# Routing between an attention and its experts: first row fetch moved into the attention's program, a weight split moved ahead, extra identity transposes on TensorE

## Chip, core and metric

The kernel runs on one core of one Trainium2 chip. The metric is device time in microseconds (us), the median of several executions. Engines: TensorE (PE in the profile; PEld is its weight load), VectorE (DVE), ScalarE (ACT), GpSimd (POOL) and SyncE (SP).

## What is computed

An attention over 4 x 12 heads of 448 tokens feeds a layer of 8 experts in which every token goes to one expert only, and that feeds a dense gated layer:

```python
x = attention(q, k, v, g_q, g_k)                  # 1792 tokens x 768
logits = (x / (|x| + 1e-6)) @ en.T / tau          # en: normed embeddings of 8 experts
expert_idx = np.argmax(logits, axis=1)
gate_w = softmax(logits)[arange, expert_idx]
for e in range(8):
    mask = expert_idx == e
    out[mask] = gate_w[mask, None] * (relu(x[mask] @ w1[e]) @ w2[e])
return (sigmoid(out @ w_gate) * (out @ w_val)) @ w_out
```

## The kernel before

The kernel is three programs in a row: `attention`, `experts` and `layer2`. Each is a block in which every engine has a list of instructions of its own in the order written, with semaphores between engines. [...]

**Routing, the end of the attention.** Tokens lie in 16 tiles of 112 rows (`TILES`); 12 are "early" (the first three batches), 4 are "late". For the late tiles VectorE picks the best expert (`best`), TensorE counts with two small products (`count`), and VectorE's `ranks` turns the counts into a slot for each token: prefix sum, subtract, add, mask, reduce, and four small steps that give the slot's chunk `r.a` and its line `r.b`. `chunk_of(i)` and `line_of(i)` write one-hot matrices HI and LO for tile i, and `index_map` multiplies LO by HI on TensorE, in all 16 products that add up in one bank: the token number of every slot. VectorE then copies that bank to `c.index` (the rows of the first job), `c.indices` (all rows, as integers) and `c.tokens` (the same as floats). In between it finishes the gates: GpSimd raises the squared norms to the power 0.5 (L520), VectorE adds 1e-6, inverts, scales the logits, ScalarE takes the exponential, and SyncE writes the gates to DRAM beside x (`write_gate`, L314).

**Experts.** Work is cut into jobs of up to 294 tokens of one expert. A job fetches its rows by three indirect DMAs of 98 rows from GpSimd (`fetch_rows`, parts a = 0, 1, 2), multiplies them by their gates (`scale_rows` on VectorE for a = 0 and 2, `scale` on ScalarE for a = 1), turns them on TensorE into six banks, and splits them into a high and a low part, XH by ScalarE and XL by VectorE (`x_out`). Each layer product is then three products (high x high, low x high, high x low). `h(j, f)` is block f of the hidden layer, 18 products; its weight block needs its low part W1L from VectorE (`w1_split`), whose high part W1H comes from ScalarE. There are two buffers, so W1H of block f can only be written when h of block f - 2 is done. W1H of blocks 0 and 1 is made already in the attention's program. Before its first job, VectorE also computes the table of jobs (`job_table`, L1444 to L1470), clears the ends of six banks, copies the turned slot table for SyncE (`tokens_T`, L1476), and, after the six `x_out`, makes the low parts of seven weight slots of layer 2 (L1512).

Of the kernel before, what the change touches and what calls it, by code (L numbers as in the profile page):

```python
# [22 lines left out]
F32 = mybir.dt.float32  # L23
# [8 lines left out]
NT = 4  # L32
# [6 lines left out]
E = 8  # L39
# [144 lines left out]
def attention(nc, c, q, k, v, g_q, g_k, emb, tau, w1, w2, w_l2, w_sums, x_rows):  # L184
# [5 lines left out]
    with ExitStack() as ctx:  # L190
# [208 lines left out]
        def _(pool):  # L399
# [120 lines left out]
            nc.gpsimd.tensor_tensor(r.norm[:, EARLY:], r.ssq[:, EARLY:], r.half[:, EARLY:], ALU.pow).then_inc(r.norm_pow, 1)  # L520
        @block.vector
        def _(dve):
# [129 lines left out]
            def ranks(tiles, OH, mask, incl, place, before, rest, tot):  # L652
# [12 lines left out]
                chain(nc.vector.tensor_scalar(r.y[:, tiles], r.r[:, tiles], 1.0 / LINES, 0.5 / LINES - 0.5,  # L665
                                              ALU.mult, ALU.add))
                chain(nc.vector.tensor_scalar(r.y[:, tiles], r.y[:, tiles], ROUND, None, ALU.add))
                chain(nc.vector.tensor_scalar(r.a[:, tiles], r.y[:, tiles], ROUND, None, ALU.subtract))
# [22 lines left out]
            def early_ranks():  # L691

                dve.wait_ge(r.counted_e, 1)
                ranks(early, r.OHE, r.mask_e, r.incl_e, r.place_e, r.cap, tqk[:, 0:E * EARLY],
                      tqk[:, E * EARLY:2 * E * EARLY]).then_inc(r.ranked_e, 1)
                only(nc.vector.tensor_tensor(r.carry[:, :], r.cap[:, :], r.incl_e[:, :, EARLY - 1], ALU.add))
# [24 lines left out]
            def finish():  # L721
# [20 lines left out]
                ranks(late, r.OHL, r.mask_l, r.incl_l, r.place_l, r.carry, sc[1][:, 0, 0:E * NT],  # L742
                      sc[1][:, 0, E * NT:2 * E * NT]).then_inc(r.ranked_l, 1)
                dve.wait_ge(r.norm_pow, 1)
                chain(nc.vector.tensor_scalar(r.norm[:, late], r.norm[:, late], 1e-6, None, ALU.add))
                chain(nc.vector.reciprocal(r.norm[:, late], r.norm[:, late]))
                nc.vector.tensor_tensor(r.L[:, late, :], r.L[:, late, :],
                                        r.norm[:, late].unsqueeze(2).to_broadcast(over_e), ALU.mult).then_inc(r.exp_in, 1)
                dve.wait_ge(r.ranked_l, 1)
# [13 lines left out]
                nc.vector.tensor_copy(c.tokens[:, :], sc[0][0:ROWS, 1, 0:SLOTS]).then_inc(c.all_indices, 1)  # L763
# [104 lines left out]
        def _(pe):  # L868
# [190 lines left out]
            count(r.OHL, sc[1][:, 0, 0:E * NT], sc[1][:, 0, E * NT:2 * E * NT], E * NT, r.counted_l)  # L1059
            index_map(range(EARLY, TILES)).then_inc(r.mapped, 1)  # L1060
# [18 lines left out]
def fetch_rows(nc, c, x_rows):  # L1079

    for a in range(GATHERS):
        nc.gpsimd.indirect_dma_start(out=c.xr[:, a, :], out_offset=None, in_=x_rows[:, :],
                                     in_offset=bass.IndirectOffsetOnAxis(ap=c.index[:, a:a + 1], axis=0))\
            .then_inc(c.x_got[a], 16)
# [108 lines left out]
def experts(nc, c, w1, w2, w_l2, w_sums, x_rows, table_of_slots, ids):  # L1193
# [4 lines left out]
    with ExitStack() as ctx:  # L1198
# [22 lines left out]
        slots_written = sem("slots_written")  # L1221
        tokens_T = sb("tokens_T", [HALF, 2, LINES], U32)
# [115 lines left out]
        def _(pool):  # L1338
# [8 lines left out]
            for ring in range(2):  # L1347
                pool.wait_ge(c.x_written[ring], 16 * PAIRS // 2)
            pool.wait_ge(c.gate_written, 16 * B)
            pool.wait_ge(c.first_index, 1)  # L1350
            fetch_rows(nc, c, x_rows)
# [3 lines left out]
            pool.wait_ge(c.all_indices, 2)  # L1355
# [18 lines left out]
        def _(act):  # L1374
# [21 lines left out]

            for k in range(7):
                nc.scalar.activation(c.WH[:, k, :], first_slot(k), ACT.Copy).then_inc(c.w_hi, 1)
# [18 lines left out]
        def _(dve):  # L1417
# [55 lines left out]
            for bank in hb + yb:  # L1473
                nc.vector.memset(bank[:, TS:T], 0.0).then_inc(banks_set, 1)
            dve.wait_ge(tokens_turned, 2)
# [29 lines left out]
            for f in range(2):  # L1505
                w1_split(0, f)
            scale_rows(0, 2)
            for kd in range(KD):
                x_out(0, kd, first_banks[kd])
            for k in range(7):  # L1510
                dve.wait_ge(c.w_hi, k + 1)
                nc.vector.tensor_tensor(c.WL[:, k, :], first_slot(k), c.WH[:, k, :].bitcast(F32),  # L1512
                                        ALU.subtract).then_inc(c.w_lo, 1)
# [4 lines left out]
        def _(pe):  # L1518
# [48 lines left out]

            n_jobs = jobs(pe, pe.wait_ge)
            pe.wait_ge(banks_set, HB + YB)
            for part in range(2):  # L1570
                nc.tensor.transpose(hb[2][0:HALF, part * 128:part * 128 + LINES],
                                    c.tokens[0:LINES, part * HALF:(part + 1) * HALF],
                                    c.ident[0:LINES, 0:LINES]).then_inc(tokens_turned, 1)
            pe.wait_ge(tokens_out, 1)
            for a in range(GATHERS):
                pe.wait_ge((gated_dve, gated_act)[a % 2], a // 2 + 1)
                for kd in range(KD):
                    last = nc.tensor.transpose(first_banks[kd][:, a * R:(a + 1) * R], xr[0:R, a, kd * 128:(kd + 1) * 128],
                                               c.ident[0:R, 0:R])
                    if a == GATHERS - 1:  # L1580
                        last.then_inc(x_turned, 1)
# [539 lines left out]
```

## Time and profile before

| | us |
|---|---|
| median of 3 runs | 1154.52 (1153.01 to 1155.78) |
| the profiled execution's own time | 1155.25 |
| span of its trace | 1153.8 |

The trace is one execution. Its span starts with the first instruction; 1.45 us of the device time lie outside it. Times in the rows below are us from the span's start. [...] Busy time of TensorE says little about its speed, since a product at the low clock is busy for twice as long.

### The profile page before, as it was taken

To read this page: it belongs to the slowest core of one execution; us is meant where nothing else is said; L and a number is where in the kernel's file an instruction comes from. 1 tells how busy PE (TensorE), PEld (TensorE's weight loads), DVE (VectorE), ACT (ScalarE), POOL (GpSimd) and SP (SyncE) were. 2 spreads that over 40 slices of the span, in tenths; PEclk is the share of its full clock that TensorE was granted. 3 is DMA by queue.
4 is the path that set the end of the run, shared out by engine and by line. 5 is a ranking of instruction groups with operands and counts; after the bars stand their busy time and mean duration, and the time that the engine had idled before them with its cause. 6 is when DMAs were issued, how large, how long until landed. Compare 5 with 4: busy or idle time off the path is not lost. (4 is left out here: it accounts for less than half of the span.)

```text
span 1153.8 us, 21938 instructions
## 1 busy us (share of the span) xinstructions
PE 1104.7 (96%) x7312; PEld 978.3 (85%) x7313; DVE 779.7 (68%) x1416; ACT 597.4 (52%) x1414; POOL 365.0 (32%) x363
## 2 busy tenths in 40 slices
PE   7999999999959899999999899999999999999997
PEld 6566666666649899999999899999999999999997
DVE  5789988788677545565556796475568675574672
ACT  4777777777625555565555663242245343341441
POOL 7798887888421110111011501100003012000002
PEclk9999999999959999999999999999999999999999
DMA  4355565543427667786778433142231334331312
GB/s 124 90 154 146 171 197 142 150 118 104 130 66 200 162 188 180 189 220 170 183 196 218 120 104 102 50 123 76 82 111 56 110 99 150 108 104 48 111 42 96
DMA packets 207779, 149.64 MB, mean 130 GB/s; under 512 B 12446, under 2 KB 203550, under 8 KB 207718
## 3 DMA queue, kind: packets, MB, share of 16 engines
q1 hardware_dynamic: 203910, 133.80, 42.1%
q0 software_dynamic: 3568, 14.82, 4.2%
q8 instruction: 36, 0.59, 0.2%
q10 hardware_dynamic: 240, 0.23, 0.1%
q14 instruction: 25, 0.20, 0.1%
HBM read 128.29 MB, written 20.53 MB: 129 GB/s over the span
## 5 line engine op out<-in xcount | busy, mean ns | idle before, releaser
L1984 PE MATMUL qb<-BH,l_WH 128*128 128x448 f32 x504 | 185.9, 369 | 3.0 <-DVE BL L1854 3.0
L1986 PE MATMUL qb<-BH,l_WL 128*128 128x448 f32 x504 | 185.9, 369 | 0.0
L1985 PE MATMUL qb<-BL,l_WH 128*128 128x448 f32 x504 | 185.9, 369 | 0.0
L1689 ACT ACTIVATE l_WH<-stream 128x384 fp32r<-128x384 f32 x209 | 100.8, 515 | 127.4 <-PE ob L2007 102.4
L1925 POOL TENSOR_TENSOR quads<-quads 128x448 f32<-128x448 f32 x24 | 30.6, 1276 | 381.7 <-DVE quads L1793 381.7
L1793 DVE TENSOR_TENSOR quads<-qb,quads 128x448 f32<-128x448 f32 x168 | 100.1, 619 | 67.6 <-PE qb L1986 67.4
L1789 DVE TENSOR_TENSOR l_WL<-stream,l_WH 128x384 fp32r<-128x384 f32 x209 | 121.3, 599 | 20.4 <-ACT l_WH L1689 20.4
L791 ACT ACTIVATE PR<-sc,negmax 112x448 f32<-112x448 f32 x192 | 121.9, 658 | 0.7 <-DVE negmax L533 0.5
L1539 PE MATMUL hb<-XH,W1H 128*128 128x256 f32 (+1 forms) x384 | 112.7, 294 | 7.4 <-issue 4.0
L1539 PE MATMUL yb<-HH,W2H 128*128 128x256 f32 (+1 forms) x384 | 112.8, 294 | 0.4 <-DVE W2L L1480 0.4
L2005 PE MATMUL ob<-l_WH,GH 128*128 128x384 f32 x336 | 112.5, 335 | 0.4 <-DVE Y L1873 0.4
L533 DVE TENSOR_REDUCE negmax<-sc 112x2 f32<-112x896 f32 x96 | 100.6, 1085 | 17.6 <-PE sc L914 17.0
L2007 PE MATMUL ob<-l_WH,GL 128*128 128x384 f32 x336 | 112.3, 334 | 0.0
L2006 PE MATMUL ob<-l_WL,GH 128*128 128x384 f32 x336 | 112.2, 334 | 0.0
L1541 PE MATMUL hb<-XH,W1L 128*128 128x256 f32 (+1 forms) x384 | 111.7, 291 | 0.0
L1540 PE MATMUL hb<-XL,W1H 128*128 128x256 f32 (+1 forms) x384 | 111.5, 290 | 0.0
L1540 PE MATMUL yb<-HL,W2H 128*128 128x256 f32 (+1 forms) x384 | 109.8, 286 | 0.0
L1541 PE MATMUL yb<-HH,W2L 128*128 128x256 f32 (+1 forms) x384 | 109.7, 286 | 0.0
L1984 PEld LDWEIGHTS qb<-BH,l_WH 128*128 128x128 f32 x504 | 95.1, 189 | 12.3 <-issue 3.2
L1423 DVE TENSOR_TENSOR W1L<-raw,W1H 128x384 fp32r<-128x384 f32 x132 | 67.9, 556 | 51.9 <-ACT W1H L1379 43.7
L1986 PEld LDWEIGHTS qb<-BH,l_WL 128*128 128x128 f32 x504 | 95.0, 189 | 9.4
L1985 PEld LDWEIGHTS qb<-BL,l_WH 128*128 128x128 f32 x504 | 95.0, 189 | 9.1
(251 smaller groups left out, 2536.1 us busy)
## 6 DMA issues: line engine op xcount, KB each, us to landing
raw<-in_moe_w_dram SPq DMA_DIRECT2D x68, 384.0 KB, 5.1
stream<-in_moe_w_dram SPq DMA_DIRECT2D x48, 512.0 KB, 5.1
stream<-w_sums SPq DMA_DIRECT2D x92, 192.0 KB, 2.4
w_sums<-Sb SPq DMA_DIRECT2D x12, 768.0 KB, 6.3
stream<-in_moe_w_out_dram SPq DMA_DIRECT2D x48, 192.0 KB, 2.4
stream<-in_moe_w_val_dram SPq DMA_DIRECT2D x36, 192.0 KB, 3.0
stream<-in_moe_w_gate_dram SPq DMA_DIRECT2D x33, 192.0 KB, 2.6
raw<-in_q_dram SPq DMA_DIRECT2D x24, 224.0 KB, 3.3
```

Of the source, the lines that this page charges most:

```text
L791: nc.scalar.activation(PR[:, h, j, :], sc[j % 2][0:P, h, 0:S], ACT.Exp, bias=negmax[:, s, j, h:h + 1], accum_out=den[:, s, h, j:j + 1]).th ...
L1539: nc.tensor.matmul(out[:, 0:n], WH[:, slot, k, :], mh, start=(k == 0), stop=False)
L1540: nc.tensor.matmul(out[:, 0:n], WH[:, slot, k, :], ml, start=False, stop=False)
L1541: last = nc.tensor.matmul(out[:, 0:n], WL[:, slot, k, :], mh, start=False, stop=(k == blocks - 1))
L1689: nc.scalar.activation(W(c.WH, n), c.stream[:, n % RING, :], ACT.Copy).then_inc(c.w_hi, 1)
L1789: nc.vector.tensor_tensor(W(c.WL, n), c.stream[:, n % RING, :], W(c.WH, n).bitcast(F32), ALU.subtract).then_inc(c.w_lo, 1)
L1984: nc.tensor.matmul(bank, wh, bh, start=(k == 0), stop=False)
L1985: nc.tensor.matmul(bank, wh, bl, start=False, stop=False)
L1986: mm = nc.tensor.matmul(bank, wl, bh, start=False, stop=(k == 2))
L2005: nc.tensor.matmul(bank, GH[:, f, at], W(c.WH, slot), start=(f == 0), stop=False)
L2006: nc.tensor.matmul(bank, GH[:, f, at], W(c.WL, slot), start=False, stop=False)
L2007: mm = nc.tensor.matmul(bank, GL[:, f, at], W(c.WH, slot), start=False, stop=(f == 3))
```

## The change

- GpSimd's fetch of part 0 for job 0 moves from the start of the experts' program to the end of the attention's (`fetch_rows(..., range(1))`), with its waits for the written rows, gates and index. Parts 1 and 2 stay in the experts' program.
- In the late tiles' ranks, the three steps on the norms (add, reciprocal, multiply) stand between the rank steps instead of behind them.
- `c.tokens` is copied by ScalarE at the start of the experts' program, no longer by VectorE at the end of the attention's.
- On VectorE, W1L of block 0 and the low part of weight slot 0 stand ahead of the `tokens_T` copy, and slots 1 and 2 stand ahead of the six `x_out`.
- TensorE gets identity transposes that nobody reads (`keep_busy`): 24 ahead of the last four index products, 40 at the start of the experts' program, 6 behind the token transposes and 4 ahead of each part's row transposes.

```diff
@@ -518,6 +518,12 @@
             nc.gpsimd.tensor_scalar(gsum, gsum, 1e-9, None, ALU.add).then_inc(r.gsum_e, 1)
             pool.wait_ge(r.ssq_l, 1)
             nc.gpsimd.tensor_tensor(r.norm[:, EARLY:], r.ssq[:, EARLY:], r.half[:, EARLY:], ALU.pow).then_inc(r.norm_pow, 1)
+            for ring in range(2):
+                pool.wait_ge(c.x_written[ring], 16 * PAIRS // 2)
+            pool.wait_ge(c.gate_written, 16 * B)
+            pool.wait_ge(c.first_index, 1)
+            fetch_rows(nc, c, x_rows, range(1))
+
         @block.vector
         def _(dve):
             nc.vector.memset(power[:, :], -0.5).then_inc(fixed, 1)
...
@@ -662,10 +668,13 @@
                                               before[:, :].unsqueeze(2).to_broadcast(wide), ALU.add))
                 chain(nc.vector.tensor_tensor(place[:, :, :], place[:, :, :], OH[:, :, :], ALU.mult))
                 chain(nc.vector.tensor_reduce(r.r[:, tiles], place[:, :, :].rearrange("p e i -> p i e"), AX.X, ALU.add))
-                chain(nc.vector.tensor_scalar(r.y[:, tiles], r.r[:, tiles], 1.0 / LINES, 0.5 / LINES - 0.5,
-                                              ALU.mult, ALU.add))
-                chain(nc.vector.tensor_scalar(r.y[:, tiles], r.y[:, tiles], ROUND, None, ALU.add))
-                chain(nc.vector.tensor_scalar(r.a[:, tiles], r.y[:, tiles], ROUND, None, ALU.subtract))
+            def over_lines(tiles):
+
+                return nc.vector.tensor_scalar(r.y[:, tiles], r.r[:, tiles], 1.0 / LINES, 0.5 / LINES - 0.5,
+                                               ALU.mult, ALU.add)
+
+            def line_in_chunk(tiles):
+
                 return nc.vector.scalar_tensor_tensor(out=r.b[:, tiles], in0=r.a[:, tiles], scalar=-float(LINES),
                                                       in1=r.r[:, tiles], op0=ALU.mult, op1=ALU.add)
 
...
@@ -739,13 +752,17 @@
                 chain(nc.vector.tensor_tensor(r.L[:, late, :], r.LG[:, late, :],
                                               r.mx[:, late].unsqueeze(2).to_broadcast(over_e), ALU.subtract))
                 dve.wait_ge(r.counted_l, 1)
-                ranks(late, r.OHL, r.mask_l, r.incl_l, r.place_l, r.carry, sc[1][:, 0, 0:E * NT],
-                      sc[1][:, 0, E * NT:2 * E * NT]).then_inc(r.ranked_l, 1)
+                numbers(late, r.OHL, r.mask_l, r.incl_l, r.place_l, r.carry, sc[1][:, 0, 0:E * NT],
+                        sc[1][:, 0, E * NT:2 * E * NT])
                 dve.wait_ge(r.norm_pow, 1)
-                chain(nc.vector.tensor_scalar(r.norm[:, late], r.norm[:, late], 1e-6, None, ALU.add))
-                chain(nc.vector.reciprocal(r.norm[:, late], r.norm[:, late]))
+                only(nc.vector.tensor_scalar(r.norm[:, late], r.norm[:, late], 1e-6, None, ALU.add))
+                chain(over_lines(late))
+                only(nc.vector.reciprocal(r.norm[:, late], r.norm[:, late]))
+                chain(nc.vector.tensor_scalar(r.y[:, late], r.y[:, late], ROUND, None, ALU.add))
                 nc.vector.tensor_tensor(r.L[:, late, :], r.L[:, late, :],
                                         r.norm[:, late].unsqueeze(2).to_broadcast(over_e), ALU.mult).then_inc(r.exp_in, 1)
+                chain(nc.vector.tensor_scalar(r.a[:, late], r.y[:, late], ROUND, None, ALU.subtract))
+                line_in_chunk(late).then_inc(r.ranked_l, 1)
                 dve.wait_ge(r.ranked_l, 1)
                 chunk_of(EARLY).then_inc(r.hi_l, 1)
                 line_of(EARLY).then_inc(r.lo_l, 1)
@@ -760,7 +777,6 @@
                 dve.wait_ge(r.mapped, 1)
                 nc.vector.tensor_copy(c.index[:, :], sc[0][0:ROWS, 1, 0:GATHERS]).then_inc(c.first_index, 1)
                 nc.vector.tensor_copy(c.indices[:, :], sc[0][0:ROWS, 1, 0:SLOTS]).then_inc(c.all_indices, 1)
-                nc.vector.tensor_copy(c.tokens[:, :], sc[0][0:ROWS, 1, 0:SLOTS]).then_inc(c.all_indices, 1)
 
             sums(0, 0, 0)
             sums(0, 0, 1)
@@ -1057,6 +1073,7 @@
             index_map(range(EARLY // 2, EARLY))
             pe.wait_ge(r.picked_l, 1)
             count(r.OHL, sc[1][:, 0, 0:E * NT], sc[1][:, 0, E * NT:2 * E * NT], E * NT, r.counted_l)
+            keep_busy(sc[1][:, 1, :], 24)
             index_map(range(EARLY, TILES)).then_inc(r.mapped, 1)
 
 
...
@@ -1344,15 +1362,11 @@
                 nc.gpsimd.dma_start(ids[bass.ds(s, T), :].rearrange("(a l) o -> a (l o)", l=LINES),
                                     table_of_slots[bass.ds(slot, GATHERS), :]).then_inc(ids_out, 16)
 
-            for ring in range(2):
-                pool.wait_ge(c.x_written[ring], 16 * PAIRS // 2)
-            pool.wait_ge(c.gate_written, 16 * B)
-            pool.wait_ge(c.first_index, 1)
-            fetch_rows(nc, c, x_rows)
+            fetch_rows(nc, c, x_rows, range(1, GATHERS))
             n_jobs = jobs(pool, pool.wait_ge)
             pool.wait_ge(slots_written, 16)
             store_ids(0)
-            pool.wait_ge(c.all_indices, 2)
+            pool.wait_ge(c.all_indices, 1)
             with pool.Fori(0, n_jobs) as j:
                 pool.wait_ge(x_turned, KD * (j + 1))
                 pool.wait_ge(ids_out, 16 * (j + 1))
@@ -1394,6 +1408,8 @@
 
                 nc.scalar.activation(HH[:, f, :], hb[f % HB][:, 0:T], ACT.Relu).then_inc(h_hi, 1)
 
+            act.wait_ge(c.all_indices, 1)
+            nc.scalar.activation(c.tokens[:, :], c.indices[:, :], ACT.Copy).then_inc(tokens_copied, 1)
             for k in range(7):
                 nc.scalar.activation(c.WH[:, k, :], first_slot(k), ACT.Copy).then_inc(c.w_hi, 1)
             n_jobs = jobs(act, act.wait_ge)
@@ -1472,6 +1488,14 @@
             job_table()
             for bank in hb + yb:
                 nc.vector.memset(bank[:, TS:T], 0.0).then_inc(banks_set, 1)
+            w1_split(0, 0)
+
+            def slot_low(k):
+                dve.wait_ge(c.w_hi, k + 1)
+                nc.vector.tensor_tensor(c.WL[:, k, :], first_slot(k), c.WH[:, k, :].bitcast(F32),
+                                        ALU.subtract).then_inc(c.w_lo, 1)
+
+            slot_low(0)
             dve.wait_ge(tokens_turned, 2)
             nc.vector.tensor_copy(tokens_T[:, :, :], hb[2][0:HALF, 0:256].rearrange("p (h l) -> p h l", h=2)[:, :, 0:LINES])                .then_inc(tokens_out, 1)
             def w2_split(j, d, part):
@@ -1502,15 +1526,14 @@
                     scale_rows(j, a)
 
             scale_rows(0, 0)
-            for f in range(2):
-                w1_split(0, f)
+            w1_split(0, 1)
             scale_rows(0, 2)
+            slot_low(1)
+            slot_low(2)
             for kd in range(KD):
                 x_out(0, kd, first_banks[kd])
-            for k in range(7):
-                dve.wait_ge(c.w_hi, k + 1)
-                nc.vector.tensor_tensor(c.WL[:, k, :], first_slot(k), c.WH[:, k, :].bitcast(F32),
-                                        ALU.subtract).then_inc(c.w_lo, 1)
+            for k in range(3, 7):
+                slot_low(k)
             with dve.Fori(0, n_jobs) as j:
                 job_order(w1_split, w2_split, h_out, scale, x_out, lambda j, d: None, j)
 
@@ -1565,14 +1588,23 @@
                     if d + 1 < KD:
                         turn(j + 1, d + 1)
 
+            def keep_busy(bank, turns):
+
+                for _ in range(turns):
+                    nc.tensor.transpose(bank[:, 0:128], c.ident[:, :], c.ident[:, :])
+
+            keep_busy(tx[0], 40)
             n_jobs = jobs(pe, pe.wait_ge)
             pe.wait_ge(banks_set, HB + YB)
+            pe.wait_ge(tokens_copied, 1)
             for part in range(2):
                 nc.tensor.transpose(hb[2][0:HALF, part * 128:part * 128 + LINES],
                                     c.tokens[0:LINES, part * HALF:(part + 1) * HALF],
                                     c.ident[0:LINES, 0:LINES]).then_inc(tokens_turned, 1)
+            keep_busy(hb[0], 6)
             pe.wait_ge(tokens_out, 1)
             for a in range(GATHERS):
+                keep_busy(hb[0], 4)
                 pe.wait_ge((gated_dve, gated_act)[a % 2], a // 2 + 1)
                 for kd in range(KD):
                     last = nc.tensor.transpose(first_banks[kd][:, a * R:(a + 1) * R], xr[0:R, a, kd * 128:(kd + 1) * 128],
```

Where the instructions stand now, at three places.

TensorE at the end of the attention, from the fourth index product group to the barrier, before (sc0 holds the index bank, sc1 the counts):

```order
L1038 MATMUL sc0<-HI,LO 112x168 [waits hi_e1,lo_e] x6
L1023 MATMUL sc1<-OHL,tri 112x32 [waits picked_l]
L1024 MATMUL sc1<-OHL,ones 112x32
L1038 MATMUL sc0<-HI,LO 112x168 [waits hi_l,lo_l] x4
L190 UNCONDITIONAL_BRANCH
L1517 UNCONDITIONAL_BRANCH [waits barrier_Pool_Activation_PE_DVE_SP_release]
```

and of the change:

```order
L1054 MATMUL sc0<-HI,LO 112x168 [waits hi_e1,lo_e] x6
L1039 MATMUL sc1<-OHL,tri 112x32 [waits picked_l]
L1040 MATMUL sc1<-OHL,ones 112x32
L890 MATMUL sc1<-ident 128x128 x24
L1054 MATMUL sc0<-HI,LO 112x168 [waits hi_l,lo_l] x4
L190 UNCONDITIONAL_BRANCH
L1540 UNCONDITIONAL_BRANCH [waits barrier_Pool_Activation_PE_DVE_SP_release]
L1594 MATMUL tx0<-ident 128x128 x40
```

The 24 transposes stand between the counts and the last four index products, and 40 more stand first in the experts' program, ahead of TensorE's load of the job table.

GpSimd from its last routing step over the barrier, before:

```order
L518 TENSOR_SCALAR gsum<-gsum 112x12 [waits pool_pick]
L520 TENSOR_TENSOR norm<-ssq,half_ 112x4 [waits ssq_l]
L190 UNCONDITIONAL_BRANCH
L1337 UNCONDITIONAL_BRANCH [waits barrier_Pool_Activation_PE_DVE_SP_gather]
L1082 DMA xr<-x_rows,index 112x769 [waits gate_written,first_index,x_written1,x_written0]
L1082 DMA xr<-x_rows,index 112x769 x2
L1256 TENSOR_LOAD table [waits table_ready]
```

and of the change:

```order
L518 TENSOR_SCALAR gsum<-gsum 112x12 [waits pool_pick]
L520 TENSOR_TENSOR norm<-ssq,half_ 112x4 [waits ssq_l]
L1099 DMA xr<-x_rows,index 112x769 [waits gate_written,first_index,x_written1,x_written0]
L190 UNCONDITIONAL_BRANCH
L1355 UNCONDITIONAL_BRANCH [waits barrier_Pool_Activation_PE_DVE_SP_gather]
L1099 DMA xr<-x_rows,index 112x769 x2
L1274 TENSOR_LOAD table [waits table_ready]
```

The DMA with the four waits now stands ahead of the barrier (the branch that waits for the other engines), and two DMAs behind it.

VectorE in the experts' program, from the last clearing of a bank to the first two low parts of x, before:

```order
L1474 MEMSET yb2 128x38
L1476 CAST tokens_T<-hb2 84x196 [waits tokens_turned]
L1256 TENSOR_LOAD table [waits table_ready]
L1256 ISA x2
L1497 TENSOR_SCALAR xr<-xr 98x768 [waits x_got0]
L1423 TENSOR_TENSOR W1L<-raw1,W1H 128x384 [waits w1_hi] x4
L1497 TENSOR_SCALAR xr<-xr 98x768 [waits x_got2]
L1485 TENSOR_TENSOR XL<-tx0,XH 128x294 [waits x_hi]
L1485 TENSOR_TENSOR XL<-tx1,XH 128x294 [waits x_hi]
```

and of the change:

```order
L1490 MEMSET yb2 128x38
L1439 TENSOR_TENSOR W1L<-raw1,W1H 128x384 [waits w1_hi] x2
L1495 TENSOR_TENSOR l2_WL<-raw0,l2_WH 128x384 [waits l2_w_hi]
L1500 CAST tokens_T<-hb2 84x196 [waits tokens_turned]
L1274 TENSOR_LOAD table [waits table_ready]
L1274 ISA x2
L1521 TENSOR_SCALAR xr<-xr 98x768 [waits x_got0]
L1439 TENSOR_TENSOR W1L<-raw1,W1H 128x384 [waits w1_hi] x2
L1521 TENSOR_SCALAR xr<-xr 98x768 [waits x_got2]
L1495 TENSOR_TENSOR l2_WL<-raw0,l2_WH 128x384 [waits l2_w_hi]
L1495 TENSOR_TENSOR l2_WL<-Sb,l2_WH 128x384 [waits l2_w_hi]
L1509 TENSOR_TENSOR XL<-tx0,XH 128x294 [waits x_hi]
L1509 TENSOR_TENSOR XL<-tx1,XH 128x294 [waits x_hi]
```

Two of the four W1L halves and one layer 2 slot moved ahead of the tokens_T copy, and two more slots stand between the scaling of part 2 and the first XL. In the lists above the layer 2 slots are l2_WL, with 7 of them behind XL before and 4 now.

## Rows read from the trace of the kernel before

**Rows 1.** The page: busy time, share of the span, instructions.
```profile
PE 1104.7 (96%) x7312; PEld 978.3 (85%) x7313; DVE 779.7 (68%) x1416; ACT 597.4 (52%) x1414; POOL 365.0 (32%) x363
```

**Rows 2.** Windows: stretch, length, busy of each engine, PEclk, DMA, GB/s.
```profile
320.00:330.00 10.00, 6.86 (x32) 6.09 (x32) 7.77 (x37) 1.79 (x10) 2.20 (x6) 0.57 0.18 24
330.00:335.00 5.00, 0.38 (x2) 0.00 (x0) 3.54 (x17) 3.00 (x7) 2.15 (x2) 0.50 0.14 27
```

**Rows 3.** Windows of TensorE alone: stretch, length, busy, PEclk, DMA, GB/s.
```profile
348.60:348.70 0.10, 0.10 (x3) 0.87 0.00 0
...
389.50:389.60 0.10, 0.10 (x2) 0.57 0.00 0
```

**Rows 4.** Timeline of the attention's end: start, length, engine, line [idle before].
```profile
323.53 4.91 SPq L314 DMA_DIRECT2D x_rows<-gate  x4
...
323.76 0.56 PE L1024 MATMUL sc<-OHL,ones 112*112 112x32 f32 x2
...
327.41 2.97 PE L1038 MATMUL sc<-HI,LO 112*112 112x168 f32 x8 [3.09 <-DVE LO L714]
...
328.36 1.56 PEld L1038 LDWEIGHTS sc<-HI,LO 112*112 112x112 f32 x6 [0.50 <-DVE LO L714]
...
328.90 0.33 DVE L714 TENSOR_SCALAR LO<-lines,line,token 112x112 f32<-112x112 f32 x1
```

**Rows 5.** DMA issues from 318 to 345 us: size, us to landing.
```profile
x_rows<-gate SPq DMA_DIRECT2D x4, 1.8 KB, 2.1
xr<-x_rows,index POOLq DMA_INDIRECT x3, 4.9
```

**Rows 6.** Timeline over the barrier to the first product of the experts.
```profile
330.42 0.16 DVE L761 CAST index<-sc 112x3 uint32<-112x3 f32 x1 [1.12 <-PE sc L1038]
...
330.74 0.32 DVE L763 COPY tokens<-sc 112x168 f32<-112x168 f32 x1
331.37 0.94 ACT L1398 ACTIVATE l_WH<-raw 128x384 fp32r<-128x384 f32 x2 [4.21 <-PEq L190]
331.86 0.16 DVE L1444 TENSOR_TENSOR_SCAN vals<-ones,cnt 1x8 f32<-1x8 f32 x1 [0.80 <-PEq L190]
...
332.32 1.23 POOL L1082 DMA_INDIRECT xr<-x_rows,index  x1 [7.83 <-issue]
...
336.39 0.18 DVE L1474 MEMSET yb<- 128x38 f32 x3
...
337.74 0.36 DVE L1476 CAST tokens_T<-hb 84x196 uint32<-84x196 f32 x1 [1.17 <-PE hb L1571]
...
338.70 0.62 DVE L1497 TENSOR_SCALAR xr<-xr 98x768 f32<-98x768 f32 x1 [0.60 <-issue]
...
339.23 1.96 DVE L1423 TENSOR_TENSOR W1L<-raw,W1H 128x384 fp32r<-128x384 f32 x4
...
341.11 0.61 DVE L1497 TENSOR_SCALAR xr<-xr 98x768 f32<-98x768 f32 x1
...
342.69 0.84 DVE L1485 TENSOR_TENSOR XL<-tx,XH 128x294 fp32r<-128x294 f32 x2 [0.97 <-ACT XH L1390]
...
343.20 0.58 PE L1539 MATMUL hb<-XH,W1H 128*128 128x256 f32 x1 [0.19 <-DVE XL L1485]
```

**Rows 7.** Timeline of the first hidden blocks of job 0.
```profile
345.86 1.95 DVE L1512 TENSOR_TENSOR l_WL<-Sb,l_WH 128x384 fp32r<-128x384 f32 x4
...
348.20 1.02 DVE L1423 TENSOR_TENSOR W1L<-raw,W1H 128x384 fp32r<-128x384 f32 x2
...
350.12 1.01 POOL L1082 DMA_INDIRECT xr<-x_rows,index  x1 [0.86 <-POOL index L1360]
350.18 0.94 ACT L1379 ACTIVATE W1H<-raw 128x384 fp32r<-128x384 f32 x2 [1.39 <-PE hb L1541]
```

**Rows 8.** Timeline: identity transposes near the start, and TensorE after its one long stop.
```profile
11.34 1.26 PE L874 MATMUL tpb<-ident 128*128 128x128 f32 x10
...
385.86 0.38 PE L1539 MATMUL hb<-XH,W1H 128*128 128x256 f32 x1 [4.04 <-issue]
```

More of the change, by code:

```diff
@@ L650, in chain, with numbers @@
                 dve.wait_ge(r.dve, n_dve[0])
-            def ranks(tiles, OH, mask, incl, place, before, rest, tot):
+            def numbers(tiles, OH, mask, incl, place, before, rest, tot):
                 W = E * (tiles.stop - tiles.start)
@@ L693, in early_ranks @@
                 dve.wait_ge(r.counted_e, 1)
-                ranks(early, r.OHE, r.mask_e, r.incl_e, r.place_e, r.cap, tqk[:, 0:E * EARLY],
-                      tqk[:, E * EARLY:2 * E * EARLY]).then_inc(r.ranked_e, 1)
+                numbers(early, r.OHE, r.mask_e, r.incl_e, r.place_e, r.cap, tqk[:, 0:E * EARLY],
+                        tqk[:, E * EARLY:2 * E * EARLY])
+                chain(over_lines(early))
+                chain(nc.vector.tensor_scalar(r.y[:, early], r.y[:, early], ROUND, None, ALU.add))
+                chain(nc.vector.tensor_scalar(r.a[:, early], r.y[:, early], ROUND, None, ALU.subtract))
+                line_in_chunk(early).then_inc(r.ranked_e, 1)
                 only(nc.vector.tensor_tensor(r.carry[:, :], r.cap[:, :], r.incl_e[:, :, EARLY - 1], ALU.add))
@@ L1076, in w2_block, with fetch_rows @@
     return w[:, :, d * 128:(d + 1) * 128]
-def fetch_rows(nc, c, x_rows):
-    for a in range(GATHERS):
+def fetch_rows(nc, c, x_rows, parts=range(GATHERS)):
+    for a in parts:
         nc.gpsimd.indirect_dma_start(out=c.xr[:, a, :], out_offset=None, in_=x_rows[:, :],
@@ L1221, in experts @@
         slots_written = sem("slots_written")
+        tokens_copied = sem("tokens_copied")
         tokens_T = sb("tokens_T", [HALF, 2, LINES], U32)
```

## Prediction

> **What bounds the kernel now.** I read the page first: TensorE is busy for 96% of the span [rows 1]. So time is lost only where TensorE stops or runs slowly. [...] Then I followed the timeline backwards from the experts' first product, at 343.20. It waits for VectorE's first XL, this for ScalarE's XH, this for the row transposes of part 2, and these for the scaling of part 2, which VectorE does at 341.11, right behind its four W1L halves [rows 6]. Further back VectorE is busy with the job table from 331.86 on, with two waits only: 1.17 ahead of the tokens_T copy and 0.60 behind it [rows 6]. The chain on the path is therefore VectorE's list, from the barrier to the XLs. The rows fetched from DRAM are not on it: part 1 is asked for at about 333.9, lands 4.9 later at about 338.7 [rows 5, 6], and is needed only while VectorE is still at its W1L halves; part 2 is scaled when VectorE gets to it.
>
> **What the path is worth.** Behind the first product, t0, comes a second limit. Before, h of blocks 0 and 1 run mostly at the low clock, 343.20 to about 349.9: ScalarE's W1H of block 3, which waits for the end of block 1, starts at 350.18 [rows 7], and TensorE goes straight on. If the clock is high instead, h(0) takes the six XLs' pace (0.42 each by [rows 6]) and about 2.4 in all; ScalarE starts W1H of block 2 at t0 + 2.6. VectorE meanwhile has six XLs (1.9 after t0) and its four remaining layer 2 slots, 0.49 each (1.95 for four, [rows 7]), so it is free at t0 + 3.9. Its W1L of block 2 (1.02, [rows 7]) ends at t0 + 4.9. h(1) would end at t0 + 4.5, so block 2 starts at t0 + 4.9. Before it starts at 349.9. The change breaks even at t0 = 345.0 and gains what t0 comes earlier than that. From there on TensorE is the bound in both and the gain is kept to the end.
>
> **The change, part by part.**
> *24 transposes ahead of the last index products.* Ten such transposes took 1.26 with a tail of 0.3 in the modelled end, so one costs 0.107 at the high clock [rows 8] and twice that, 0.213, at the low one. They start when the counts are issued, at about 324.1 [rows 4]: all at the low clock they end at 329.0. The index products could begin at 327.4 before [rows 4]. One is two records of 0.28 at the low clock (six loads in 1.56, [rows 4], with some wait), 0.56, and 0.28 at the high one. How soon the clock rises under steady work has two rows: product work from 343.20 to 348.6 is 5.4, and from 385.86 to 389.5 is 3.7 [rows 3, 6, 8]. TensorE is busy for 6.86 of the ten from 320, with 2.97 of it from 327.41 [rows 2, 4], so nearly all of 320.5 to 324.3 is work already, and the clock may rise anywhere from about 325 to 329.5. With a rise at 328 the transposes end at 328.6 and four products at 329.9, against 330.4 before: 0.5 earlier. With one at 325 VectorE's last LO, at 329.2 less 0.2, is the limit, and the end is 329.4. With no rise before the end it is 329.0 + 4 x 0.56 + 0.25, 331.5. I take 329.9, as the middle of the three.
> *Norms among the rank steps.* Three steps of VectorE of 0.2 each now start without waiting for the step ahead of them. That makes HI and LO of the first late tile ready some 0.2 earlier and the exponential's input 0.4 earlier. Both go under the transposes; at zero cover they gain 0.2. The gates' last DMA was issued at about 327.9 and lands 2.1 later, 330.0 [rows 4, 5]; it comes up to 0.3 earlier.
> *First fetch ahead of the barrier.* GpSimd needs the index copy (0.2 behind the index products: 330.1) and the gates (about 329.9). In the loop a fetch starts 0.86 behind the copy that releases it [rows 7], so it starts at about 331.0 and is issued in 1.23 [rows 6], until 332.2. GpSimd is the engine that releases the barrier. Before, the last to arrive was VectorE with the tokens copy, at 331.06 [rows 6]. So everything behind the barrier starts about 1.1 later: VectorE's table at 333.0, TensorE at 332.5. GpSimd's own second and third fetch come 1.1 after the release, at 333.3 and 334.6, against 333.9 and 335.1; they gain 0.5, and nobody on the path wants them. What is bought, part 0 fetched 1.3 earlier, is off the path. Bounds for this term: 0 (the release doesn't wait for the fetch) and 1.6 (the fetch waits for a late gate).
> *Tokens copy to ScalarE.* VectorE leaves the attention 0.24 earlier, hidden by GpSimd. ScalarE pays about 0.3 ahead of its seven WH copies (0.47 each, from 331.37 on, [rows 6]); they would end near 336, and the first of them that VectorE wants is wanted at 338.7. Nothing.
> *VectorE's new order.* From the last memset, 336.57, to the first XL, 342.69, it was 6.12 [rows 6]. Now the list is: two W1L halves 0.98, slot 0.49, tokens_T 0.36, table load 0.60, scaling 0.62, two halves 0.98, scaling 0.61, two slots 0.98. That is 5.6, in which the turning and ScalarE's XH for part 2 (0.97) hide under the two slots. It gains 0.5, and three slots less stand behind t0, which is in the break-even above.
> *40 transposes at the experts' entry.* They begin at 332.5. TensorE has then been idle for 2.6, and before it was idle for 3 between 324.4 and 327.4 with the clock low on both sides. From the low clock, with a rise 3.7 to 5.4 later, 40 end at 338.6 to 339.4, and the token transposes 0.4 later. VectorE wants them at 337.7 + 1.5 = 339.2. So it waits 0 to 0.7; with the clock high at entry they end at 336.8, and it does not wait at all. I take 0.4.
> *The small groups of 6 and 4* fill TensorE's waits for VectorE's scalings, 0.4 to 0.6 each at the high clock, where it waits 0.6 to 1.0. At the low clock a group of four is 0.85, which can put 0.3 on the path. What they are for is that the clock is high at t0; I count on it.
>
> **Sum.** t0 = 343.2 + 1.1 (barrier) - 0.5 (VectorE's order) + 0.4 (wait for the tokens) = 344.2. Against 345.0 that gains 0.8: the change earns about 2.6 by the clock and gives most back, in the barrier above all. The profiled execution took 1155.25, of which 1153.8 are the span; it becomes 1154.45. The median of the runs shown is 0.73 below that execution, so I predict 1153.7.
>
> [...]
>
> **Rivals.**
> *A: the release does not wait for the fetch.* The loop shows the fetch's start and length, but no row shows whether the barrier's instruction passes GpSimd while the fetch is being issued. Then the barrier comes at about 330.7 instead of 332.2, even 0.4 earlier than before, and with 0.4 for the tokens t0 is 342.5 to 343.0. The gain is 2.0 to 2.5: 1152.0 to 1152.5. Against it: the release stands behind the fetch in GpSimd's list. [...]
> *B: the transposes come too late in the clock.* If the clock has not risen when the 24 end, at 329.0, the index products end at 331.5, 1.1 later than before and 1.6 later than in my sum; t0 becomes 345.8, and the change loses 0.8, with a late rise in the 40 as well 1.5: 1155.3 to 1156.0. It decides from a rise later than about 329 on. For it: the clock was still low at 343.20, behind the row transposes [rows 2, 3]. Against: both rises came within 5.4 of steady work.
> *C: the clock is lost in the small waits.* h(0) and h(1) then run at the low clock as before, block 2 starts at t0 + 6.6 = 350.8, and the change loses 0.9: 1155.4. It needs the waits to outweigh the fillers, which are as long as most of them.
>
> **Chances.** My sum 0.57, A 0.23, B 0.13, C 0.07. The runs before differ by up to 2.8, and what a measurement here can tell from no change is about 0.2%, 2.3 us. Half of A and a little of my sum lie beyond it on the fast side, for which both of its uncertain terms must fall away, the barrier's 1.1 and the 0.4 at the tokens: 0.19. On the slow side there is only the end of B with a late clock at entry: 0.06. The likeliest gives 1153.7; A's end at 1151.9 and B's at 1156.0 bound the range.
>
> **What would show it.** In the profile of the changed kernel: the fetch of part 0 starting 0.8 to 0.9 behind the index copy, and ScalarE's first instruction of the experts only behind its end (right: barrier term; wrong: A). PEclk above 0.5 before the last four index products (wrong: B). The token transposes starting as the 40 end, with VectorE waiting for them 0 to 0.7. t0 at 344.2 with PEclk 1.0 through h(0) (wrong: C), and block 2 waiting for VectorE's W1L. The prediction fails if the fetch's rows turn out to be on the path, or if block 2 doesn't wait, so that the full 2.6 of the clock comes through.

## The result: slower, and the profile after

The changed kernel takes 1156.94 us in the median of 11 runs (1154.79 to 1162.84), the kernel before 1154.53 of 11 (1151.59 to 1156.49). The ratio is 1.0032, interval 1.002 to 1.0045: slower, by 3.7 us at the ratio; the two medians alone lie 2.4 apart. I had said 1153.7, 0.8 faster, with 1156.0 as the upper end.

The profiled execution has a span of 1158.5, against 1153.8. The page's line on busy time, which answers to [rows 1], says nothing of the cause:

```profile
PE 1114.3 (96%) x7394; PEld 987.5 (85%) x7395; DVE 784.3 (68%) x1415; ACT 598.6 (52%) x1415; POOL 364.9 (31%) x363
```

The windows do; the first answers to the first of [rows 2] and the others lie around the barrier (stretch, length, busy PE, PEld, DVE, ACT, POOL, PEclk, DMA, GB/s). PEclk is the granted clock of TensorE as a share of full speed; I call 0.50 the low clock and 1.00 the high one. Before, it was 0.57 from 320 to 330 and 0.50 from 330 to 335 [rows 2], and 0.87 in the slice at 348.6 [rows 3].

```profile
320.00:330.00 10.00, 8.57 (x51) 7.86 (x50) 8.56 (x40) 1.79 (x10) 3.42 (x9) 0.74 0.17 25
...
334.00:335.00 1.00, 0.00 (x0) 0.00 (x0) 0.00 (x0) 0.00 (x0) 0.80 (x1) 0.97 0.00 0
335.00:336.00 1.00, 0.00 (x0) 0.00 (x0) 0.00 (x0) 0.00 (x0) 0.43 (x1) 0.50 0.00 0
336.00:337.00 1.00, 0.00 (x0) 0.00 (x0) 0.00 (x0) 0.00 (x0) 0.00 (x0) 0.50 0.81 160
337.00:338.00 1.00, 0.00 (x0) 0.00 (x0) 0.00 (x0) 0.00 (x0) 0.00 (x0) 0.50 0.45 185
```

From 336 to 338 no engine does anything, while DMA engines are busy for 0.81 and 0.45 of the time, at 160 and 185 GB/s. The timeline of the same stretch and of what follows, which answers to [rows 6, 7, 8] (start, length, engine, line, what, and the idle time before it with its releaser):

```profile
331.73 1.30 PE L1054 MATMUL sc<-HI,LO 112*112 112x168 f32 x8
...
333.08 0.16 DVE L778 CAST index<-sc 112x3 uint32<-112x3 f32 x1 [1.30 <-PE sc L1054]
...
334.20 1.23 POOL L1099 DMA_INDIRECT xr<-x_rows,index  x1 [7.07 <-DVE index L778]
338.66 0.34 ACT L1412 ACTIVATE tokens<-indices 112x168 f32<-112x168 uint32 x1 [9.44 <-PEq L190]
...
338.98 5.91 PE L1594 MATMUL tx<-ident 128*128 128x128 f32 x40 [5.94 <-PEq L190]
339.15 0.16 DVE L1460 TENSOR_TENSOR_SCAN vals<-ones,cnt 1x8 f32<-1x8 f32 x1 [5.67 <-PEq L190]
...
339.29 0.95 POOL L1099 DMA_INDIRECT xr<-x_rows,index  x1 [3.87 <-POOLq L190]
...
343.71 0.18 DVE L1490 MEMSET yb<- 128x38 f32 x3
...
344.74 0.54 DVE L1495 TENSOR_TENSOR l_WL<-raw,l_WH 128x384 fp32r<-128x384 f32 x1
...
345.20 0.34 DVE L1500 CAST tokens_T<-hb 84x196 uint32<-84x196 f32 x1
...
349.41 0.83 DVE L1509 TENSOR_TENSOR XL<-tx,XH 128x294 fp32r<-128x294 f32 x2 [0.34 <-ACT XH L1404]
...
349.93 0.39 PE L1562 MATMUL hb<-XH,W1H 128*128 128x256 f32 x1 [0.58 <-DVE XL L1509]
...
390.71 0.58 PE L1562 MATMUL hb<-XH,W1H 128*128 128x256 f32 x1 [4.15 <-issue]
```

The fetch is issued by 335.43, and the first engine enters the experts' program at 338.66. The DMA issues of that fetch give its landing, 4.1 from its start, so 338.3:

```profile
xr<-x_rows,index POOLq DMA_INDIRECT x1, 4.1
```

In the lists of both kernels GpSimd has the barrier's wait for `gather` and TensorE its wait for `release`. The traces show this of it: in all twelve profiles of this study no engine has an instruction of the experts' program before VectorE's last copy of the attention has ended: before, that is at 331.06, and ScalarE starts at 331.37; in the changed kernel it is at 333.47, and ScalarE starts at 338.66. And in e4 (below), where GpSimd alone works until 340.29, ScalarE starts at 341.20, TensorE at 341.52 and VectorE at 341.69.

Times from a trace's start can't be compared directly. The norm power L520, GpSimd's last routing step, starts at 323.45 before and at 326.10 in the change, though TensorE, VectorE and the others have the same work up to there in both. All that follows is therefore counted from L520. The table has every profile of this study; "job 1" is the start of TensorE's first product of job 1, behind its one long stop, and the last column is what lies between the first product and it.

| profile | index copy | VectorE enters | first product | job 1 | job 1 less first product |
|---|---|---|---|---|---|
| before | 6.97 | 8.41 | 19.75 | 62.41 | 42.66 |
| after | 6.98 | 13.05 | 23.83 | 64.61 | 40.78 |
| e1_fetch_back | 6.70 | 7.90 | 18.51 | 59.75 | 41.24 |
| e2_fetch_only | 6.57 | 13.46 | 24.83 | 67.64 | 42.81 |
| e3_no_drain | 6.50 | 8.11 | 19.15 | 60.01 | 40.86 |
| e4_pool_work | 6.75 | 14.95 | 26.25 | 67.27 | 41.02 |
| e5_order_alone | 6.42 | 7.62 | 18.68 | 60.91 | 42.23 |
| e6_turns_alone | 5.87 | 7.08 | 18.70 | 61.25 | 42.55 |
| e7_no_24 | 6.79 | 7.99 | 19.24 | 60.05 | 40.81 |
| e8_three_fetches | 6.79 | 16.69 | 28.84 | 69.95 | 41.11 |
| e9_back_no_drain | 6.89 | 8.17 | 18.78 | 60.14 | 41.36 |
| e10_before_no_drain | 6.95 | 8.47 | 19.83 | 61.91 | 42.08 |

The change itself is worth +2.2 in the profiles at job 1 (64.61 - 62.41). The other 2.65 by which the two profiles differ up to L520 belongs to the attention ahead of it, and I don't count it to the change: the three profiles with the attention of before reach L520 at 323.45, 324.82 and 328.75, and the nine with that of the change at 324.52 to 332.72, so the two ranges overlap.

### The profile page after: what moved, and what is told of

Its sections match the earlier page's. It is cut to its first block and busy times, and to the rows that moved or that the text cites. A ratio compares the mean times of both kernels' runs of the same rounds, so it can differ in the third digit from the quotient of the medians.

```text
span 1158.5 us, 22103 instructions
## 1 busy us (share of the span) xinstructions
PE 1114.3 (96%) x7394; PEld 987.5 (85%) x7395; DVE 784.3 (68%) x1415; ACT 598.6 (52%) x1415; POOL 364.9 (31%) x363
```

## Experiments

### The fetch put back, alone, or without the drain

Three theories, all of them guesses, were set against each other. D: GpSimd's part in the barrier waits until its own DMA has landed (in the changed kernel it lands at 338.3, and the first engine enters at 338.66). C: it is not the landing, but a load of GpSimd's next program that comes behind a fetch. P: my sum was right about the barrier and something else of the change costs the time. With "the drain" I mean what the argument `no_gpsimd_drain=True` takes away from a block. The word is the argument's; the traces list no such instruction, and show only when the engines enter with it and without.

**e1_fetch_back**, the changed kernel with

```diff
-            fetch_rows(nc, c, x_rows, range(1))
...
-            fetch_rows(nc, c, x_rows, range(1, GATHERS))
+            fetch_rows(nc, c, x_rows)
```

(the first of these lines in the attention's program, the others in the experts', to which the four waits ahead of the fetch go back too).

> The changed kernel with all three fetches of job 0 back in the experts' program; everything else of the change stays. Times are told from GpSimd's norm power ahead of the barrier (323.45 before, 326.10 in the changed kernel); from there VectorE enters the experts' program after 8.4 before and 13.05 in the change, and the first product starts after 19.75 and 23.8. Theory D (at the end of its block GpSimd waits until its own outstanding DMA has landed, and the barrier waits for GpSimd): entry back at 8.2 to 8.4, first product at 19.3, some 2 us faster than before, ratio 0.998. Theory C (GpSimd's next program has to be loaded behind a fetch) says the same of this run. Theory P (my sum was right about the barrier and the loss is made by the transposes and the new order): first product stays above 21.5 and the run is not faster than before.

Measured: 1155.73 against 1158.59 for the kernel before beside it, ratio 0.9977 (0.996 to 0.9994). Faster, by 2.7 at the ratio and 2.66 at job 1. Everything of the change but the fetch gains; P is out. VectorE enters at 7.90, a little earlier than the 8.2 to 8.4 of D.

**e2_fetch_only**, the kernel before with the opposite of that diff.

> The kernel before with only the fetch of part 0 moved ahead of the barrier. D and C: VectorE enters the experts' program some 4.6 later than before (13.0 behind GpSimd's norm power), nothing gives it back, ratio 1.004, 1159. P: at most 1.1 later, ratio 1.001.

Measured: ratio 1.0042 (1.0022 to 1.0062), 4.9 us; VectorE enters 13.46 behind L520, job 1 comes 5.2 later. The fetch alone costs all that the changed kernel lost, and more.

**e3_no_drain**, the changed kernel, fetch ahead of the barrier, with

```diff
-        block = ctx.enter_context(nc.Block())
+        block = ctx.enter_context(nc.Block(no_gpsimd_drain=True))
```

> The changed kernel, with the attention's block closed without GpSimd's drain instruction. D: the barrier no longer waits for the landing; VectorE enters the experts' program 8.3 to 9.4 behind GpSimd's norm power, the first product comes at 19.3 to 20.3, and the run is 1.3 to 2.2 us faster than the kernel before (ratio 0.998 to 0.999). C: the drain has nothing to do with it, entry stays at 13.0 and the time near 1157, ratio 1.002 to 1.003.

Measured: ratio 0.9975 (0.9956 to 0.9993), entry 8.11, job 1 2.4 earlier than before. D had 8.3 to 9.4 for the entry. C is out: with the same fetch in the same place the entry is at 8.11 without the drain and at 13.05 with it. The timeline of this kernel shows how:

```profile
331.24 0.16 DVE L778 CAST index<-sc 112x3 uint32<-112x3 f32 x1 [0.56 <-PE sc L1054]
...
332.35 0.34 ACT L1412 ACTIVATE tokens<-indices 112x168 f32<-112x168 uint32 x1 [4.22 <-PEq L190]
...
332.36 1.23 POOL L1099 DMA_INDIRECT xr<-x_rows,index  x1 [6.58 <-POOLq L190]
```

ScalarE is already in the next program (332.35) when GpSimd's fetch begins (332.36). The barrier does not even wait for the fetch's issue, as rival A had it. A small cost is left: ScalarE enters 1.11 behind the start of the index copy, against 0.70 in e1 and 0.77 in e9. And the time is that of e1 (0.9975 and 0.9977; job 1 at 60.01 and 59.75): rows that come earlier are worth nothing here, with or without the barrier's cost.

**e4_pool_work**, the changed kernel with, behind the fetch,

```diff
+            for _ in range(4):
+                chain(nc.gpsimd.tensor_tensor(xq[:, :, :], X[:, 0, :, :], X[:, 0, :, :], ALU.mult))
```

> The changed kernel with four products of 112x512 on GpSimd (about 1.05 us each with their waits, 4.5 in all, result unused) between the fetch of part 0 and the end of the attention's block. D: the fetch lands under them, so ScalarE's first instruction of the experts comes less than 1 us behind their end, about 1.5 later than in the changed kernel. C: it comes some 3 us behind their end, as it does behind the fetch now. If GpSimd cannot start them until the fetch has landed, they start 3 us behind its issue.

It ran once, for its timeline:

```profile
334.61 1.23 POOL L1101 DMA_INDIRECT xr<-x_rows,index  x1 [6.84 <-DVE index L780]
335.88 4.41 POOL L527 TENSOR_TENSOR xq<-X 112x512 f32<-112x512 f32 x4
...
341.20 0.34 ACT L1414 ACTIVATE tokens<-indices 112x168 f32<-112x168 uint32 x1 [11.34 <-PEq L190]
```

GpSimd works on 0.04 behind the fetch's issue, so it is not held by the transfer itself; and the next program starts 0.9 behind the end of its work, 340.29, not 3. The fetch's data moved under the work: the DMA share is 0.06 from 338.0 to 338.5 and 0.00 from there to 341. So it is the end of the block that waits, and not GpSimd's next instruction. ScalarE's entry is 1.9 later than in the changed kernel, both counted from L520 (14.46 and 12.56); I had expected 1.5.

**e8_three_fetches**, the changed kernel with `fetch_rows(nc, c, x_rows)` ahead of the barrier and none behind it.

> The changed kernel with all three fetches of job 0 ahead of the barrier. If the drain waits for landings, the barrier waits for the third fetch's: VectorE enters the experts' program 2.4 to 3.0 later than in the changed kernel, 15.5 to 16.1 behind GpSimd's norm power, or about 3 behind the end of the third fetch's issue. If the drain costs a fixed time from the first fetch's issue, entry stays at 13.0 or follows the issues alone.

It, too, ran once, for its timeline:

```profile
335.20 0.93 POOL L1099 DMA_INDIRECT xr<-x_rows,index  x1 [0.30 <-issue]
...
340.71 0.34 ACT L1411 ACTIVATE tokens<-indices 112x168 f32<-112x168 uint32 x1 [13.06 <-PEq L190]
```

and, from the DMA issues, the time from the third fetch's issue to its landing:

```profile
xr<-x_rows,index POOLq DMA_INDIRECT x1, 5.1
```

The third fetch lands at 340.3 and ScalarE starts 0.4 later; with one fetch it was 338.3 and again 0.4. The wait follows the last landing, and not the last issue: behind the end of the issue it is 4.6 here (336.13 to 340.71) and 3.2 with one fetch (335.43 to 338.66). My 15.5 to 16.1 for VectorE's entry was 0.6 short, because the third fetch takes 5.1 and not 4.1 to land.

### The rest of the change, in halves

**e5_order_alone** leaves out the fetch's move and all `keep_busy` calls of the change; **e6_turns_alone** leaves out the fetch's move and puts VectorE's entry list back:

```diff
-            w1_split(0, 0)
...
-            slot_low(0)
...
-            w1_split(0, 1)
+            for f in range(2):
+                w1_split(0, f)
             scale_rows(0, 2)
-            slot_low(1)
-            slot_low(2)
...
-            for k in range(3, 7):
+            for k in range(7):
```

Two theories were set against each other: T, that the order and the clock pay only together, and S, that each pays by itself and the two add up.

> The changed kernel with the fetches back in the experts' program and without any of the added identity transposes: what is left is VectorE's new order, the norms among the rank steps and the tokens copy on ScalarE. Theory T (order and clock only pay together, because block 2 of job 0 waits for VectorE if the clock is high in the old order, and for TensorE if the clock is low in the new): first product 19.1 behind GpSimd's norm power (19.75 before, 18.5 with both), hidden blocks 0 and 1 at the low clock, job 1's first product 0.7 earlier than before (61.7, against 62.4 before and 59.75 with both), ratio 0.9994. Rival S (the parts add up, and the order is the larger): job 1 at 61.0 or less, ratio 0.9988.

> The changed kernel with the fetches back in the experts' program and VectorE's entry list in the order of before (four W1L halves between the scalings, seven layer 2 slots behind the XLs); transposes, norms and tokens copy stay. T: the clock is high at the first product, but block 2 of job 0 waits for its W1L behind seven slots, from 4.4 to 6.4 behind the first product; job 1's first product about 0.5 to 1.0 earlier than before, ratio 0.9993. S: the clock alone is worth about 2 of the 2.7, job 1 at 60.5, ratio 0.998.

Measured: order alone 0.9988 (0.9974 to 1.0002), transposes alone 0.9994 (0.998 to 1.0008). Neither can be told from no change by its time, and the two intervals don't separate T from S. Nor do the totals at job 1: e5 came at 60.91 with a ratio of 0.9988, which is what S had forecast, and e6 at 61.25 and 0.9994, which is nearer to T. From before they gain 1.50 and 1.16, and the sum, 2.66, is just what e1 gains. But e6's index copy came 1.1 earlier than before's and e5's 0.55, e1's only 0.27. Counted from the index copy on, order alone gains 0.95, the transposes alone 0.06, and both together (e1) 2.39; e10, which differs from before only by the drain, gains 0.48 in the same count, so that is the noise of one profile. The table's last column leaves out what happened ahead of the first product as well. It is 42.66, 42.81 and 42.08 in the three profiles with neither, 42.23 with the order alone, 42.55 with the transposes alone, and 40.8 to 41.4 in all seven profiles with both. So behind the first product the two pay together: 41.03 in the mean of seven against 42.52 of three, 1.5. Each alone lies within the spread of the profiles with neither, so there it pays nothing that one profile can tell. Ahead of the first product the order pays alone: from the index copy to the first product it is 12.26 in e5, 12.78 before and 12.88 in e10, so 0.5. Why the transposes alone pay so little is in e6's timeline: the clock is high (PEclk 1.00 from 346.22 to 352.20; its first W1H comes 2.6 behind the first product), and block 2 of job 0 then waits for VectorE's W1L:

```profile
346.22 0.39 PE L1557 MATMUL hb<-XH,W1H 128*128 128x256 f32 x1 [0.60 <-DVE XL L1505]
...
351.20 1.02 DVE L1438 TENSOR_TENSOR W1L<-raw,W1H 128x384 fp32r<-128x384 f32 x2
...
352.27 0.38 PE L1557 MATMUL hb<-XH,W1H 128*128 128x256 f32 x1 [1.43 <-DVE W1L L1438]
```

T's mechanism, the wait of block 2 and what the two pay together behind the first product, stands; that it is the whole account rests on single profiles and is not shown by times. T's totals at job 1 don't come out: 60.91 and 61.25 for 61.7 and 61.4 to 61.9. Both profiles came to the first product earlier than before did, by 1.07 and 1.05 (I had 0.65 for e5). In e6 nearly all of that is the index copy, 1.1 earlier.

**e7_no_24** leaves out the fetch's move and `keep_busy(sc[1][:, 1, :], 24)`.

> The changed kernel with the fetches back and without the 24 transposes ahead of the last index products; the 40, 6 and 4s stay. If the 24 help, as my sum had it, by 0.5, the last index product ends 0.3 to 0.5 later behind GpSimd's norm power than with them and the run is that much slower than with them (0.9980). If they are in the way as often as they help, there is no difference, 0.9977.

Measured: 0.9985 (0.9972 to 0.9998). Times don't tell it from e1. The copies do: with the 24 the index copy starts 5.87 to 6.98 behind L520 in seven profiles, mean 6.64; without them 6.42 to 6.97 in five, mean 6.74. So 0.1, nothing that can be told. Where the clock is high (0.98 in e3, 1.00 in e6) they end in 2.8 to 2.9 and the copy is early (e6 5.87, e3 6.50); where it is low (0.52 in the changed kernel and in e9) they take 4.9 to 5.1 and the copy is later (after 6.98, e9 6.89).

### The drain without a transfer

**e9_back_no_drain** is e1 with the attention's drain taken away as in e3, **e10_before_no_drain** the kernel before with only that.

> The changed kernel with all three fetches of job 0 back in the experts' program and the attention's block closed without GpSimd's drain. If the drain costs only what an outstanding GpSimd DMA makes it wait for, this is the same as with the fetches back alone (0.9977 to the kernel before, VectorE entering the experts' program 1.2 behind its index copy). If an idle GpSimd's drain also costs, entry comes up to 0.4 earlier and the ratio is 0.9973.

> The kernel before, with the attention's block closed without GpSimd's drain. GpSimd has no DMA of its own outstanding there. Drain waits for landings only: no difference, ratio 1.000, VectorE enters 1.44 behind the start of its index copy. Drain costs by itself: up to 0.3 us earlier, ratio 0.9997, which the time alone cannot tell but the timeline can.

Measured: 0.9978 (0.9966 to 0.999) and 0.9997 (0.9986 to 1.0008). From the index copy to VectorE's entry it is 1.28 in e9 and 1.20 in e1, 1.52 in e10 and 1.44 before. So with nothing of GpSimd's outstanding the drain costs nothing here. That it waits for landings is my reading of e2, e3, e4, e8, e9 and e10 together: with one fetch and with three ScalarE enters 0.4 behind the last landing, without the drain ahead of it.

e1, e3 and e9 beat both kernels, at 0.9975 to 0.9978 of the kernel before. e1 is the simplest of them.

## Why the prediction was wrong, point by point

**The barrier term: the step that failed.** I wrote under "First fetch ahead of the barrier" that everything behind the barrier starts about 1.1 later, with bounds of 0 and 1.6. It was 4.64 (13.05 - 8.41). What I could take from rows was right: the fetch starts 0.96 behind the end of the index copy (0.86 forecast) and is issued in 1.23. But I ended the wait with the issue. In its place stood the landing, 4.1 behind the start of the issue, plus 0.4 to ScalarE's entry, and with the drain left out (e3) neither. Rows 5 had that landing, 4.9, and I used it only for the question when the rows are there. No row of before could show the wait, since GpSimd had no transfer of its own under way at that barrier; that was a reason for a wider upper bound, not for taking the issue's end. With 3.5 more in the sum, my 0.8 faster becomes 2.7 slower.

**Who needs the rows.** Right: part 0 is off the path. e3 has it asked for with the barrier cost gone and is no faster than e1. Part 2 is off it by little: in e1 it is asked for at 335.74, lands 4.8 later at 340.54, and VectorE scales it at 340.72.

**VectorE's new order.** Forecast 0.5 from the last memset to the first XL. Measured 343.89 to 349.41, 5.52, against 6.12: 0.6.

**The tokens' wait.** Forecast 0.4, of 0 to 0.7. In the changed kernel it was nothing: the slot ends at 345.28 and the copy stands right behind it, with TensorE's token transposes at 344.73. That it was nothing is luck of the clock: the 40 transposes took 5.91 here at a mean PEclk of 0.76, and 6.18 at 0.73 in e3, which has no wait either; in e7 they took 6.39 at 0.70 and the wait was 0.33, and in e8 7.29 at 0.62 and it was 1.28, beyond my 0.7. Whether the clock would be lost at the barrier I had left open. In the changed kernel TensorE's last index product ended at 333.03, and PEclk was 0.97 from 334 to 335 and 0.50 from 335 to 336. In e1, where TensorE was idle for 1.07, it was 1.00 through all 40, which took 4.56. The sum had this term and the barrier's wrong in opposite directions, by 0.4 and 3.5.

**The break-even, 1.8 behind the old first product.** Measured 1.88 (42.66 - 40.78). With it the profile's result follows: 4.64 - 0.6 + 0 = 4.04 later at the first product (4.08 measured), less 1.88, 2.2 slower. Block 2 waits for VectorE's W1L, as forecast, but barely:

```profile
353.52 1.02 DVE L1439 TENSOR_TENSOR W1L<-raw,W1H 128x384 fp32r<-128x384 f32 x2
...
354.59 0.39 PE L1562 MATMUL hb<-XH,W1H 128*128 128x256 f32 x1
```

It starts 4.66 behind the first product, for 4.9 forecast. Behind the first product the clock and the order pay together only, and somewhat less in the mean of the profiles (1.5, above) than in this one.

**The 24 transposes.** Forecast 0.5 earlier; 0.1 in the mean of profiles, which is nothing.

**Rivals.** A's step, that the release doesn't wait for the fetch, is what happens without the drain, and its time, faster by 2.0 to 2.5, is near e3's: 2.4 at job 1, 2.9 at the ratio. Its barrier 0.4 earlier than before did not come: from the index copy to ScalarE's entry it is 1.11 in e3 and 0.95 before. In the changed kernel, with the drain, the step doesn't show: ScalarE enters 3.2 behind the end of the issue. B's mechanism, a low clock under the 24, happened in the profiled execution (they took 5.14, at 0.52) but cost nothing, since the clock had risen before the index products (1.30 for their eight records at 1.00, against 2.97 at 0.50 before). C did not happen: the granted clock is 1.00 from 342 to 352. None of the three named the landing.

**The rest of the gap.** The ratio says 3.7, interval 2.3 to 5.2, and the profiles 2.2. e2's cost (4.9) less e1's gain (2.7) is 2.2 as well, and the medians lie 2.4 apart. I take the difference for the spread of the runs; that is not shown.

## What to carry to other kernels

In this program a transfer issued by GpSimd just ahead of the attention's end put its whole landing (4.1, and 0.4 more), not its issue (1.23), ahead of what ScalarE, TensorE and VectorE do in the next block. Work of GpSimd's own behind it hid the landing (e4, entry 0.9 behind that work), and with the drain left out the wait was gone (e3, 8.11 for 13.05). Before moving an early start across such a barrier, ask what each engine must have finished there, and price the barrier by the landing. And when two limits lie close together (here TensorE's clock and VectorE's list), price the edits as a pair: behind the first product neither alone gave what a profile can tell from nothing, and both together gave 1.5 us.

## What the runs showed of the hardware beside that

The attention does the same work up to L520 in every kernel, yet it took from 323.45 to 332.72 until there. The granted clock goes with it: from 0 to 320 its mean is 0.99 in the eight profiles that reach L520 at 323.45 to 326.74, and 0.98, 0.98, 0.97 and 0.96 in e6, e2, e9 and e5, at 327.52, 328.75, 329.82 and 332.72. Near the start, in the windows of before, the changed kernel and e2, whose L520 is at 323.45, 326.10 and 328.75:

```profile
20.00:40.00 20.00, 16.98 (x126) 12.10 (x127) 14.46 (x20) 13.69 (x37) 16.42 (x14) 0.91 0.21 62
...
20.00:40.00 20.00, 16.24 (x110) 11.54 (x108) 12.59 (x18) 13.16 (x35) 14.20 (x12) 0.83 0.25 69
...
20.00:40.00 20.00, 16.34 (x98) 13.12 (x96) 11.16 (x15) 11.86 (x32) 14.36 (x13) 0.69 0.23 68
```

As an estimate from these, 20 us at 0.83 in place of 0.91 are 1.6 us of TensorE's work, of the 2.65 between the first two. In e5 the clock was low for long later on (windows as above):

```profile
280.00:290.00 10.00, 7.70 (x54) 5.47 (x51) 6.67 (x15) 5.92 (x17) 9.69 (x11) 0.87 0.01 2
290.00:300.00 10.00, 10.00 (x43) 6.46 (x42) 3.24 (x5) 4.01 (x12) 0.67 (x1) 0.50 0.54 153
```

and in e1, at the same place, not at all:

```profile
280.00:290.00 10.00, 8.48 (x60) 5.15 (x62) 6.48 (x15) 7.04 (x22) 8.41 (x8) 1.00 0.02 5
290.00:300.00 10.00, 9.55 (x80) 6.68 (x78) 7.21 (x11) 6.84 (x20) 1.80 (x2) 1.00 0.69 201
```

In ten microseconds TensorE issued 43 products at the low clock, busy for all ten, and 80 at the high one, busy for 9.55. So one profile against one profile can't show an effect of 2 us in this kernel unless it is read from a common event near the change. TensorE's stop ahead of job 1, 3.9 to 4.5 in every profile with no releaser in the trace, stays unexplained.
